# A linear-attention and two-MLP kernel on one core: expert weights asked for on SyncE's queue, dispatch pairs one chunk sooner, last outputs ahead of turning

## The reference

```python
# 1: attention with complex decay; B=4, H=8, S=768, D=48
mag = np.sqrt(a_re * a_re + a_im * a_im)
scale = np.minimum(mag, 0.999) / (mag + 1e-06)
for t in range(S):
    S_re, S_im = ar * S_re - ai * S_im + kv_t, ar * S_im + ai * S_re
    y[:, :, t] = einsum('bhd,bhde->bhe', q[:, :, t], S_re)
# 2: soft mixture of 8 experts, 4 slots each; N=3072 tokens, D=384, F=1024
logits = x @ phi
d = softmax over the tokens;  slot_input = d.T @ x
slot_out[e] = np.maximum(slot_input[e] @ w1[e], 0) @ w2[e]
c = softmax over the slots;   x = c @ slot_out
# 3: MLP, 384 -> 2048 -> 384
h = np.maximum(x @ w_in, 0);  out = h * h @ w_out
```

## Time and profile before

| | us |
|---|---|
| median of three runs | 705.66 (704.86 to 709.02) |
| the profiled execution, own time | 709.5 |
| its span in the profile | 707.8 |
| PE busy in the span | 529.5 (75%) |
| DVE busy | 403.1 (57%) |
| ACT busy | 327.2 (46%) |
| POOL busy | 157.9 (22%) |

### The profile page before, as it was taken

The page is one execution under the profiler, slowest core; times in us unless marked ns, Lnnn a source line. Parts: engine busy times, 40 slices in busy tenths (PEclk is TensorE's granted clock), DMA queues, the critical chain, the costliest instruction groups (busy, mean ns, idle before and its releaser), DMA issues.

```text
span 707.8 us, 11711 instructions
## 1 busy us (share of the span) xinstructions
PE 529.5 (75%) x4544; PEld 401.9 (57%) x4544; DVE 403.1 (57%) x661; ACT 327.2 (46%) x555; POOL 157.9 (22%) x131
## 2 busy tenths in 40 slices
PE   1000009796597975969787987897999999999997
PEld 1000006575375754657576863445888888888885
DVE  1399995899699996969643315034333323333331
ACT  4867043363655826313132341244565655565553
POOL 5001000100001000010000000057555555555553
PEclk9999999898699988979898999999999999999999
DMA  6030082553636333668799696920010100000011
GB/s 237 2 132 0 2 213 65 114 123 80 196 96 131 106 80 79 129 196 252 134 237 263 137 426 260 425 103 1 2 45 1 44 2 34 11 15 31 1 45 44
DMA packets 39558, 79.59 MB, mean 112 GB/s; under 512 B 7120, under 2 KB 28752, under 8 KB 37200
## 3 DMA queue, kind: packets, MB, share of 16 engines
q1 hardware_dynamic: 36192, 62.33, 31.0%
q10 hardware_dynamic: 3312, 16.52, 7.1%
HBM read 55.12 MB, written 4.72 MB: 85 GB/s over the span
## 4 chain that ended last, share of the span: by engine, by line
PE 48%; DVE 21%; DMA 10%; ACT 7%; SPq 5%; issue 5%; POOL 3%; ACTq 0%; DVEq 0%; POOLq 0%
PE ps L1200 9%; PE ps L1202 9%; PE ps L1201 9%; PE ps L954 7%; DMA stk<-xout 7%; SPq L248 4%; DMA wouts<-in_w_out 3%; PE ps L1184 3%; PE ps L940 2%; DVE tt L666 2%; DVE xout L762 2%; DVE big L671 2%; DVE tt L668 2%; SPq L258 2%; PE ps L994 2%
## 5 line engine op out<-in xcount | busy, mean ns | idle before, releaser
L924 DVE TENSOR_TENSOR qs<-rs 128x512 f32<-128x512 f32 x96 | 70.0, 730 | 147.7 <-ACT rs L548 147.7
L613 POOL TENSOR_TENSOR hlo<-qs,hhi 128x512 fp32r<-128x512 f32 x96 | 124.7, 1300 | 92.4 <-DVE qs L924 89.4
L940 PE MATMUL ps<-ident 128*32 128x512 bf16 x260 | 76.0, 399 | 90.6 <-DMA stk<-xout 90.6
L954 PE MATMUL ps<-stk 112*128 112x224 f32 (+1 forms) x384 | 92.7, 408 | 54.2 <-DMA stk<-xout 38.3
L954 PEld LDWEIGHTS ps<-stk 112*128 112x128 f32 x384 | 82.0, 236 | 66.3 <-DMA stk<-xout 43.2
L1200 PE MATMUL ps<-hhi,who 128*128 128x512 f32 x288 | 112.8, 392 | 4.0 <-POOL hlo L613 4.0
L1202 PE MATMUL ps<-hhi,wlo 128*128 128x512 f32 x288 | 112.5, 391 | 0.0
L1201 PE MATMUL ps<-hlo,who 128*128 128x512 f32 x288 | 112.5, 391 | 0.0
L548 ACT ACTIVATE rs<-ps 128x512 f32<-128x512 f32 x96 | 57.4, 598 | 95.6 <-PE ps L1184 95.4
L940 PEld LDWEIGHTS ps<-ident 128*32 128x32 bf16 x260 | 21.0, 98 | 113.0 <-DMA stk<-xout 90.9
L598 POOL MEMSET big<- 128x2304 f32 x4 | 8.1, 2037 | 286.1 <-DVE big L671 286.1
(11 more groups left out here) (146 smaller groups left out, 825.8 us busy)
## 6 DMA issues: line engine op xcount, KB each, us to landing
stk<-xout SPq DMA_DIRECT2D x144, 128.0 KB, 3.7
wt<-in_w SPq DMA_DIRECT2D x10, 1536.0 KB, 11.9
xq<-in_xq SPq DMA_DIRECT2D x24, 384.0 KB, 4.8
wt<-in_w ACTq DMA_DIRECT2D x6, 1536.0 KB, 8.6
big<-in_a_all ACTq DMA_DIRECT2D x9, 768.0 KB, 7.1
vr<-in_v_all SPq DMA_DIRECT2D x24, 192.0 KB, 4.1
out<-ost SPq DMA_DIRECT2D x6, 768.0 KB, 3.5
wins<-in_w_in SPq DMA_DIRECT2D x1, 3072.0 KB, 17.7
```

The lines of the kernel that those rows point to most:

```text
L613: pool.tensor_tensor(hlo[:, i % NHS, :], qs[:, i % NQS, :], hhi[:, i % NHS, :].bitcast(F32), ALU.subtract).then_inc(lo_ready, 1)
L924: dve.tensor_tensor(qs[:, i % NQS, :], rs[:, i % NQS, :], rs[:, i % NQS, :], ALU.mult).then_inc(sq_ready, 1)
L940: nc.tensor.matmul(ps[P - SL:P, 7, :], idb[:, 0:SL], idle, start=True, stop=True)
L954: last = nc.tensor.matmul(ps[:, h // 2, h % 2 * SK:h % 2 * SK + cols], x[:, 0:CH], x[:, CH:CH + cols], start=True, stop=True)
```

## The change

ACT's `load_w` goes; SP asks for weight loads 0 to 5 in the same rounds, each after it has waited for the landing of that round's restack, and before that round's `xq` and `vr`. Loads 6 to 8 also wait for the last restack. The pair j moves from round 2j + 4 to round 2j + 3 on DVE, ACT and PE, with the waits that belong to it, and the loops of PE and ACT end one round sooner. `outputs(23)` and its copy move from round 24 to the end of round 23, ahead of `turn_x(22)`.

```diff
--- before.py
+++ after.py
@@ -275,6 +275,17 @@
                     n = (p - 1) * NC + c
                     if p:
                         stack(n)
+                        early = (p - B + 1) * 3 + c - (2 if p < B else 0)
+                        if p == B - 1 and 2 <= c < 5 or p == B and c < 3:
+
+                            sp.wait_ge(stacked[n % NST], 96 * (n // NST + 1))
+                            if early == 0:
+                                sp.wait_ge(an_ready, DT * B)
+                                sp.wait_ge(m_ready, 2 * B)
+                            if early == 3:
+                                sp.wait_ge(chain, C_ALL * B)
+                                sp.wait_ge(kq_ready, 2 * NC * (B - 1))
+                            load_w(early)
                         if n + NXQ < NT:
                             load_xq(n + NXQ)
                         if n > 0 and n + NV - 2 < NT:
@@ -283,10 +294,8 @@
                         stack_turns(p)
 
             sp.wait_ge(kq_ready, 2 * NT)
-            for k in range(6, 9):
-                load_w(k)
             sp.wait_ge(stacked[(NT - 1) % NST], 96 * ((NT - 1) // NST + 1))
-            for k in (10, 9):
+            for k in (6, 7, 8, 10, 9):
                 load_w(k)
             sp.wait_ge(y_done, NT)
             for k in range(11, NW):
@@ -314,10 +323,6 @@
                 dst = big[:, RAW:RAW + 2 * PF].rearrange("p (c t x) -> p c t x", c=2, t=DT)
                 act.dma_start(dst[:, :, t], a_all[b, :, :, t]).then_inc(ld_raw[t], 16)
 
-            def load_w(k):
-                src = (w2 if k % 2 else w1)[k // 2].rearrange("p a b -> p (a b)")
-                act.dma_start(wt[k][:], src).then_inc(ld_w[k], 16)
-
             def take_squares(b, t):
                 act.wait_ge(ld_raw[t], 16 * (b + 1))
                 if b:
@@ -448,7 +453,7 @@
             for t in range(DT):
                 inv_mag(0, t)
             for p in range(B + 1):
-                for c in range(NC + 3 * (p == B)):
+                for c in range(NC + 2 * (p == B)):
                     n = (p - 1) * NC + c
                     if c == 0 and p < B:
                         for t in range(DT):
@@ -456,15 +461,6 @@
                             if p < B - 1:
                                 load_raw(p + 1, t)
                         norm_squares(p)
-                    if p == B - 1 and 2 <= c < 5:
-                        if c == 2:
-                            act.wait_ge(m_ready, 2 * B)
-                        load_w(c - 2)
-                    if p == B and c < 3:
-                        if c == 0:
-                            act.wait_ge(chain, C_ALL * B)
-                            act.wait_ge(kq_ready, 2 * NC * (B - 1))
-                        load_w(3 + c)
                     if p < B - 1:
                         if c == 1:
                             for t in range(DT):
@@ -479,7 +475,7 @@
                         if c == 4:
                             for t in range(DT):
                                 inv_mag(p + 1, t)
-                    pair = n // 2 - 2 if n >= 4 and n % 2 == 0 else None
+                    pair = (n - 3) // 2 if n >= 3 and n % 2 else None
                     if pair is not None:
                         exponentials(pair)
                     if 0 <= n < NT and has_turn(n):
@@ -488,7 +484,7 @@
                         copy_flipped(2 * pair)
                     if 0 <= n < NT and has_turn(n):
                         copy_kt(n, 1)
-                    if 1 <= n <= NT:
+                    if 1 <= n < NT:
                         copy_y(n - 1)
                     if pair is not None:
                         copy_flipped(2 * pair + 1)
@@ -496,6 +492,8 @@
                         copy_state(n)
                     if pair is not None:
                         copy_sums(pair)
+                    if n == NT - 1:
+                        copy_y(n)
                     if n == NT:
                         copy_raw(n - 1)
                     if 1 <= n <= NT:
@@ -836,8 +834,8 @@
                             build_turn(n)
                     if p < B:
                         parts_in(p, lo, mid)
-                    if n >= 4 and n % 2 == 0:
-                        running_max(n // 2 - 2)
+                    if n >= 3 and n % 2:
+                        running_max((n - 3) // 2)
                     if 1 <= n <= NT:
                         apply_mask(n - 1, 0)
                         apply_mask(n - 1, 1)
@@ -1017,8 +1015,8 @@
                 pe.wait_ge(y_copied, m + 1)
                 if m:
                     pe.wait_ge(x_copied, m)
-                if m >= 3:
-                    pe.wait_ge(et_copied, (m - 1) // 2 * 2)
+                if m >= 2:
+                    pe.wait_ge(et_copied, m // 2 * 2)
                 for u in range(NU):
                     last = nc.tensor.transpose(x_ps[:, u, :], xts[0:XR, m % 2, u, :], ident[0:XR, 0:XR])
                 last.then_inc(x_done, 1)
@@ -1026,7 +1024,7 @@
             def flip(m):
 
                 pe.wait_ge(exp_done, m // 2 + 1)
-                pe.wait_ge(x_copied, min(m // 2 * 2 + 3, NT))
+                pe.wait_ge(x_copied, m // 2 * 2 + 2)
                 if m == NT - 1:
                     pe.wait_ge(raw_copied, NT)
                 elif m:
@@ -1054,15 +1052,15 @@
                 nc.tensor.matmul(ps[:, 4, k * P:(k + 1) * P], xsb[:, 0, 0:P], ident[:], start=True, stop=True)
             pe.wait_ge(stacked[0], 96)
             keep_busy(14)
-            for n in range(NT + 3):
+            for n in range(NT + 2):
                 full = n < NT - NC
-                pair = n // 2 - 2 if n >= 4 and n % 2 == 0 else None
+                pair = (n - 3) // 2 if n >= 3 and n % 2 else None
                 if n < NT:
                     keep_busy(6 if full else 1)
                     scores(n)
                 if pair is not None:
                     flip(2 * pair)
-                if 1 <= n <= NT:
+                if 1 <= n < NT:
                     keep_busy(1)
                     outputs(n - 1)
                 if pair is not None:
@@ -1073,6 +1071,8 @@
                 if pair is not None:
                     keep_busy(1)
                     weighted_sums(pair)
+                if n == NT - 1:
+                    outputs(n)
                 if n == NT:
                     logits(n - 1)
                 if 1 <= n <= NT:
```

## The result

The changed kernel takes 748.74 us (median of four runs, 747.72 to 750.37) against 707.34 for the kernel before in the same comparison: a ratio of 1.060, interval 1.0565 to 1.0636. The forecast was 741, with 722 to 757 around it. In the profiled executions the span went from 707.8 to 748.6, by 40.8 us where the walk had 35.2. Some executions of a kernel are a per cent or two slower than its others; they are left out of every ratio, and one of e4's four (767.15 us) out of its median.

A forecast was written before the change was run, and what follows sets the result against it. It saw no single bound: PE held 48% of the chain, and DVE set the pace in phases 2 and 3. 26.5 + 11 - 2.3 = +35.2 on the profiled 709.5 gave 744.7, as a median 741, range 722 to 757.

The forecast's parts named there:

- the walk: Round-by-round sum of delays against the earlier trace: +26.5 us up to scores(18), +35.2 over the whole profiled execution.
- Part 1: Pairs one chunk sooner: in odd rounds DVE's maximum waits for ACT's raw copy, +26.5 us up to scores(18).
- the slack: Rounds 3 to 5: scores(4) had waited for PE, so 3.3 us of DVE's 7.2 us delay would be absorbed.
- ACT is not late there: Moved exponentials share a table load with the logarithm in one round a phase; the pair's work costs nothing new.
- rival D: Longer gaps on PE bring half clock to five more chunks in the loop: +15 us, 756; chance 0.1.
- some 97 and 94 us instead of 85 and 87: Sign in the profile after that would show the forecast right: the lengthened durations of attention phases 2 and 3.
- Part 2: Weight loads on SP: restack 14's 4 us collision goes, restacks 15 and 16 lose about 2, phase 4 costs +11.
- rival C: Weight loads don't stand in line before restacks, so phase 4 costs 0: +24 us, 730; chance 0.2.
- Part 3: Attention's end: one round falls away and the last outputs run while ACT copies chunk 22, -2.3 us.
- I take 0: After the attention: tail loads 6 to 8, asked for 3 us later, have room; cost 0, at most 3 us.
- A: The maximum finds its raw logits there in odd rounds, so only the gains remain: 694 us; chance 0.05.
- B: After the first stall DVE and PE fall into step, later waits are short: about +14 us, 720; chance 0.13.

The follow-up runs named there:

- e4: Kernel before with one wait added: in odd rounds DVE waits, ahead of the masks, for the raw copy of the chunk before last; 758.36 us, ratio 1.076.
- e5: Changed kernel with DVE's maximum taken over a constant, without its wait for raw logits; ACT's exponentials wait instead; 719.69 us, ratio 1.021.
- e10: Changed kernel with the maximum behind the masks and the second half of DVE's scan work, ahead of the next key_query; 721.41 us, ratio 1.022.
- e1: Kernel before with only the pairs moved to odd rounds, weight loads and last outputs as before; 749.48 us, ratio 1.063.
- e7: Changed kernel with the next xq and v asked for ahead of SP's wait and weight load; 744.11 us, ratio 1.053.
- e9: Changed kernel with DVE's maximum moved behind the two masks; 742.00 us, ratio 1.050.
- e12: Changed kernel with the last outputs back in their old place; 754.02 us in a single run.
- e2: Kernel before with only the six weight loads moved to SP, behind the landed restack and in front of the next; 714.12 us, ratio 1.011.
- e3: Kernel before with only the last outputs moved ahead of the turning of chunk 22; 707.82 us, ratio 1.0014.
- e6: Kernel before with ACT's weight loads asked for after the first copy of turned keys, still on ACT's queue; 705.27 us, ratio 0.998.

## Why the prediction was right, and where its terms were off

**Part 1, the wait.** Right in mechanism and place. The maximum waited in every odd round, for over 8 us at each place c = 3, the masks followed at once, e5 and e10 bring most of the loss back by taking the wait away or covering it, and e4 shows that this wait alone costs more than the whole change. The walk's shift of the masks in round 3 was 7.2 and is 7.4. Later ones were too small: rounds 9 and 15 end their masks at 250.08 and 345.37, +23.6 and +30.5, where the walk had 19.5 and 25.4. The step that failed is the slack: "there are 3.3 us of slack and raw(3) comes only some +3.3 to +3.9". Raw(3) came 5.4 us late, and scores(4) 6.4, close behind a raw(2) that was 6.4 late as well: PE was the late one there, not the restack. Up to scores(6) the walk had 7.6 and measured are 14.5, the largest miss of all terms. "ACT is not late there" was wrong: in the changed kernel PE's flips wait 8.9 us for ACT's exponentials (2.4 before), 3.79 of them in round 3, e5 shows behind what, and e5, without DVE's wait, is 5.9 us late at scores(6), most of that miss.

The clock is a second suspect. Over the attention (113 us to the last sums) the granted clock is 0.87 of 352.2 us and was 0.90 of 313.8; added up, PE had 91 us at 1.2 GHz instead of 65. In the six traces with the full wait (after, e1, e4, e7, e9, e12) it is 85 to 99 us, in the seven without it 58 to 72, in e10 75. So longer waits on PE and more half clock go together, as rival D had it. But the price looks small: in phase 2 of e10 the granted clock was 0.85, as low as the 0.86 of the changed kernel, and the phase took 87.9 us against 95.8, and 85.2 before. What it adds where DVE waits for PE's rounds no run separates.

The sign "some 97 and 94 us instead of 85 and 87" held for phase 2 (95.8) and not for phase 3: 84.1, and the 87 was itself 7 us too long by where the earlier trace rows was cut. From scores(12) to scores(18) the walk added 7.0 and measured are 4.4.

**Part 2, the loads.** I had -4 and +2 ahead of scores(18), and +11 behind. e2 shows -7.8 and +13.3 for this part alone; in the changed kernel rounds 18 to 23 cost +9.5. The first term was mis-sized, by a factor of four for the loads alone: I counted one collision, restack 14, and in e2 the lead grows from 4.5 us at scores(14) to 7.8 at scores(18). What gives the other 3.3 no run separates. The second was near. In e1, where loads are still issued beside restacks and all waits are longer, the segment from scores(12) to (18) is 96.6; in the changed kernel it is 84.1. So the 26.5 for the way to scores(18), measured 29.6, was near only by luck, since two errors met: the pairs alone cost 39.3 there and the other parts gave 10 back. The line of 14.9 us from landing to landing was good (14.8, 15.4, 14.2; three times 14.9 are 44.7, not 44.8), and rival C falls with it. That its term of 5.2 for the restack is right by itself isn't shown; only the sum is.

The Trainium skill, "DMA: Bandwidth & Descriptors", section "Queues, rings and completion order", has each DMA engine take turns between the two queues packet by packet and take what stands in one of them in order. The runs agree in kind: a load beside a restack made its last piece take 12.89, a load in front of it 9.40 to 10.60. That the delay is by the same bytes, as the prediction put it, they do not show.

**Part 3.** The step "the 2 us of one outputs and one hand-over of 0.3" failed: it is worth 0 (e3), and what shortens the tail, 1.1 us, belongs to the pairs (e1).

**After the attention.** "I take 0" for the late loads; it was +2.1, but not through them. The DMA engines still run dry there (share 0.68, then 0.00 from 477 to 481), so no load came too late for them, and the clock is at 0.50 from 463 to 473:

```profile
463.00:467.00 4.00, 3.42 (x19) 2.02 (x18) 0.00 (x0) 1.03 (x4) 0.00 (x0) 0.51 1.03 439
467.00:470.00 3.00, 3.00 (x15) 1.75 (x19) 2.27 (x5) 0.00 (x0) 0.00 (x0) 0.50 0.99 418
470.00:473.00 3.00, 3.00 (x20) 1.44 (x16) 1.99 (x5) 0.84 (x1) 0.00 (x0) 0.50 1.04 438
473.00:477.00 4.00, 4.00 (x34) 1.39 (x26) 3.62 (x5) 0.60 (x1) 0.00 (x0) 0.96 0.68 286
477.00:481.00 4.00, 3.06 (x37) 1.48 (x36) 0.69 (x1) 0.60 (x1) 0.00 (x0) 1.00 0.00 0
```

Of the matmuls of the first four experts (L1111) 43 took 7.16 us in one piece of the chain, half of it at this clock; before, 45 took 5.31. All traces bear this out. In six (after, e1, e5, e6, e10, e12) the clock falls so around the last sums, PE has 11.2 to 14.7 us at half clock from there to the end of the span, and the rest takes 281.8 to 284.4 us; in the other eight it has 5.1 to 5.7, and the rest takes 280.8 to 281.3.

"TensorE: Matmul & The Clock Gate" of the Trainium skill, section "HAM oscillation", lets waits on PE bring the clock down. The traces don't show that for this fall. In the 30 us ahead of the last sums PE's longest standstill is 1.52 us in the changed kernel and the same in e7, where the clock stayed at 1.00 and the rest took 281.1; it is 0.97 us in e6 and e10, where the clock fell, and in the kernel before, where it didn't. Why it fell stays open.

**The sum.** In the walk's order, forecast and measured: to scores(6) 7.6 and 14.5, phase 2 11.9 and 10.6, phase 3 7.0 and 4.4, phase 4 11 and 9.5, the tail -2.3 and -0.3, the rest 0 and 2.1. The misses have both signs, and part of how near 35.2 came to 40.8 is that they cancel.

**Rivals A and B.** No maximum found its input there, so A falls. B would have had short waits after the first; they stayed at 8.34 and 8.90 in rounds 9 and 15 and were 17.36 in round 21.

## What to carry to other kernels

An operation moved one round sooner on an in-order engine costs nothing by its own 0.4 us; what counts is when its input comes, and what stands behind it. Ask that of every engine in turn: here DVE had run almost a round ahead of PE, and a wait for the end of PE's round took that lead away. If it must move, put the filler work in front of it (e10 gave back 26 of 41 us). A large load wants a moment when its queue is free and nobody waits for the next transfer; behind a landed transfer is such a moment only if the next one isn't ready yet.

## What the runs showed that I had not expected

- A wait alone (+53 us, e4) cost more than the same wait with the work that needs it moved along (+44, e1), perhaps since the move takes the work out of the rounds that everyone then waits for.
- Parts don't add: 44, 8.6 and 0 us alone, 41 together. The loads on SP cost 8.6 us in the fast kernel; with the pairs moved, loads and outputs together cost nothing that can be told from zero (+41 against +44, with overlapping intervals).
- Two small transfers (576 KB in all) in front of a restack cost 5.7 of the 7.9 us that rounds 18 to 20 lost (e7); with them moved, the next two rounds lost 3.1 again.
- Seven us of ACT work ahead of one short exponential stopped PE for 4.5 us in round 3 (e5), though ACT is busy for under half the span.
- The clock dropped at the end of the attention in the changed kernel and not in e7, with 2 us of difference in a stretch whose instructions no edit touches; the same in five more of the fourteen traces.
